# An attention and feed-forward kernel on one core: raw keys transposed two heads at a time and placed by transfers, reciprocals sent through DRAM, an order of work written out per tile, and a rearranged end of the attention part

## The chip, the cores and the metric

One core of a Trainium2 chip runs the whole kernel. The metric is the time of one execution on the device in microseconds (us), lower is better. The core has five engines with queues of their own: PE (TensorE, matmuls and transposes), ACT (ScalarE), DVE (VectorE), POOL (GpSimd) and SP (SyncE, which here issues the transfers). They wait for each other on semaphores only.

## The reference

The inputs are float32: q, k, v of 4 batches x 8 heads x 1152 rows x 64; weights of two feed-forward blocks. In attention two neighbouring query rows are averaged, so that a head has 576 query rows and 1152 keys.

```python
def _attn_ref(q, k, v):
    q_pool = q.reshape(B, H, S // 2, 2, D).mean(axis=3)
    scores = np.matmul(q_pool, k.transpose(0, 1, 3, 2)) / sqrt(D)
    attn = np.exp(scores - np.max(scores, axis=-1, keepdims=True))
    attn = attn / (np.sum(attn, axis=-1, keepdims=True) + 1e-09)
    return np.matmul(attn, v)
def _moe_ref(x, w_in, w_out):          # x: 2304 x 512, w_in: 512 x 2048
    h = x @ w_in
    g = np.where(h >= 1, h, np.where(h <= -1, 0.0, (h + 1) ** 2 / 4))
    return g @ w_out
def _moe2_ref(x, w1, w2, w3, w_out):   # 512 x 768 each
    return np.maximum(np.maximum(x @ w1, x @ w2), x @ w3) @ w_out
```

## The kernel before, in words

**Attention** goes over 16 pairs of heads, each in 9 tiles (`TILES`) of 128 query rows; the middle one (`M_TILE`) holds the last 64 rows of both heads. To keep float32 precision, operands are split into a high part (hi, rounded to the matmul's type fp32r) and a low part (lo, the rest), and products are added. Keys lie in `kT` with hi on 64 partitions and lo on the other 64, so one matmul with a doubled query sums both parts.

For a tile s these steps follow one another. *S*: PE writes scores in three groups of 384 keys (`tile_scores`), two matmuls a group (four in the middle tile), into a ring of four PSUM banks, `SCORE_RING`; a group waits (`exp_done`) until the exp of the tile that had the bank is done. *M*: DVE takes the maximum of each group, and of the three (`tile_max`). *E*: ACT makes exp in two instructions, of one and two groups (`tile_exp`). *T*: PE transposes the probabilities in three groups of three 128x128 blocks (`tile_transposes`) into a ring of three banks, `RING`. ACT copies each as pT_hi (`hi_of_tile`), DVE subtracts for pT_lo (`lo_of_tile`), which frees the bank. *V*: PE multiplies by the values in four parts a pair (n = 0 to 3: head and half), of 18 products of 288 columns each (`value_products`); the last two parts are finished in the first tiles of the next pair. ACT copies their own 64 rows to `X` and the other 64 to `value_aux`, and POOL adds them (`add_values`).

Beside that the next pairs are prepared (`PREP`). POOL splits the keys of a head into hi and lo side by side (`keys`), PE transposes 18 blocks a pair (K, six groups) and ACT copies them to `kT`. POOL adds the query pairs, PE transposes 9 blocks (Q), ACT and DVE make hi and lo. For the reciprocals of the sums (R), POOL spreads them over blocks, PE transposes five, and DVE multiplies `X` by them (`scale_x`).

The order on PE, ACT and DVE is the same row of steps in each tile: `PE_ORDER`, `ACT_ORDER` and `DVE_ORDER`, with X for the preparations of that tile. E, M and S with a number act on the next tile, N0 on the tile after it. On SP, `loads` issues the transfers of values, queries and keys, all in one queue.

**Feed-forward** goes over tiles of 384 tokens; PE makes hidden chunks (hid) and adds their products (acc), POOL splits weights into slots (`split_weights`). Three slots lie in memory that attention frees early, and are split before the last additions (`early_weights`).

## Time and profile before

| | |
|---|---|
| median of 3 runs | 1293.17 us (1292.39 to 1294.75) |
| the profiled execution | 1294.91 us, span of its trace 1293.0 us |
| granted TensorE clock, mean | 0.996 of full speed |
| busy of the span | PE 97%, DVE 59%, ACT 51%, POOL 26% |
| attention, first to last scores matmul | 12.74 to 568.22 us |
| first product of the feed-forward part's second matmul | 590.07 us |

Busy times are those of the profile; for PE they are modelled, since matmuls overlap. An idle time with an arrow names what ended it. "x3" means three instructions merged into one row.

### The profile page before, as it was taken

How to read it: one execution, taken by the hardware profiler on the slowest of the kernel's cores; microseconds unless marked ns; L12 is line 12 of the kernel's file. 1: busy time of each engine (PE TensorE's matmuls, PEld its weight loads, DVE VectorE, ACT ScalarE, POOL GpSimd, SP SyncE). 2: the span in 40 equal slices, each digit the busy share in tenths (PEclk: the TensorE clock that was granted, in tenths of full speed). 3: DMA queues.
4: the chain of work that ended last, by engine and by line, in shares of the span. 5: the costliest groups of instructions: out<-in, count | busy, mean ns of one | idle time of the engine just before them, and what ended most of it. 6: DMA issues, size and time to landing. Idle time of an engine off the chain costs nothing.

```text
span 1293.0 us, 21136 instructions
## 1 busy us (share of the span) xinstructions
PE 1259.6 (97%) x7876; PEld 1207.9 (93%) x7876; DVE 758.1 (59%) x1579; ACT 658.8 (51%) x1570; POOL 335.5 (26%) x332
## 2 busy tenths in 40 slices
PE   7999999999999999989999999999999999999998
PEld 6989899999989898979999999999999999999997
DVE  5888888888888888874544444444453222223221
ACT  5989899999989898962222222222222111111111
POOL 5343443444433444258600000000282000000000
PEclk9999999999999999989999999999999999999999
DMA  3111111111111111113300000000030000000000
GB/s 119 47 56 56 52 33 57 53 41 56 56 47 56 56 56 38 52 49 100 113 1 1 1 1 1 1 1 1 17 122 26 1 25 25 1 25 5 20 25 25
DMA packets 59140, 49.07 MB, mean 38 GB/s; under 512 B 2977, under 2 KB 48033, under 8 KB 59041
## 3 DMA queue, kind: packets, MB, share of 16 engines
q1 hardware_dynamic: 59040, 47.72, 12.1%
q8 instruction: 65, 1.06, 0.3%
q14 instruction: 35, 0.28, 0.1%
HBM read 42.99 MB, written 4.72 MB: 37 GB/s over the span
## 4 chain that ended last, share of the span: by engine, by line
PE 79%; ACT 18%; DVE 1%; issue 1%; POOL 1%; DMA 0%; SPq 0%; POOLq 0%; ACTq 0%
PE hid L868 33%; PE acc L900 16%; ACT probs L558 8%; PE trans L413 8%; ACT pT_hi L548 6%; PE acc L932 6%; PE scores L456 6%; PE values L475 5%; PE scores L458 4%; ACT kT L568 1%; ACT value_aux L582 1%; PE trans L424 1%; DVE qT L662 1%; ACT X L578 1%; ACT qT L571 1%
## 5 line engine op out<-in xcount | busy, mean ns | idle before, releaser
L626 DVE TENSOR_REDUCE neg_max_parts<-scores 128x1 f32<-128x384 f32 x432 | 234.7, 552 | 44.0 <-PE scores L458 30.3
L548 ACT ACTIVATE pT_hi<-trans 128x384 fp32r<-128x384 f32 x432 | 191.2, 491 | 55.8 <-PE trans L413 52.3
L640 DVE TENSOR_TENSOR pT_lo<-trans,pT_hi 128x384 fp32r<-128x384 f32 x432 | 212.0, 546 | 7.3 <-ACT pT_hi L548 6.3
L558 ACT ACTIVATE probs<-scores,neg_max 128x768 f32<-128x768 f32 (+1 forms) x288 | 212.0, 753 | 4.0 <-DVE neg_max L633 4.0
L456 PE MATMUL scores<-kT,qT 128*128 128x384 f32 x480 | 199.6, 416 | 9.4 <-ACT probs L558 9.1
L413 PE MATMUL trans<-ident,probs 128*128 128x128 f32 x1296 | 189.7, 273 | 9.6 <-DVE qT L662 6.4
L413 PEld LDWEIGHTS trans<-ident,probs 128*128 128x128 f32 x1296 | 157.5, 140 | 24.9 <-DVE qT L662 11.5
L868 PE MATMUL hid<-qT,w_slots 128*128 128x384 f32 x936 | 171.6, 336 | 0.0
L868 PE MATMUL hid<-x_hi,w_slots 128*128 128x384 f32 x624 | 167.6, 335 | 0.0
L868 PEld LDWEIGHTS hid<-qT,w_slots 128*128 128x128 f32 x936 | 163.7, 188 | 1.0
L986 ACT ACTIVATE excess<-rise,halves 128x384 f32<-128x384 f32 x96 | 59.2, 617 | 203.0 <-DVE rise L1070 203.0
L458 PE MATMUL scores<-kT,qT 128*128 128x384 f32 x480 | 162.2, 338 | 0.0
L900 PE MATMUL acc<-own_g,w_slots 128*128 128x384 f32 x648 | 143.1, 336 | 0.0
L900 PEld LDWEIGHTS acc<-own_g,w_slots 128*128 128x128 f32 x648 | 115.6, 188 | 0.0
L868 PEld LDWEIGHTS hid<-x_hi,w_slots 128*128 128x128 f32 x624 | 113.7, 188 | 0.6
L456 PEld LDWEIGHTS scores<-kT,qT 128*128 128x128 f32 x480 | 91.6, 191 | 23.4 <-ACT probs L558 20.1
L339 POOL TENSOR_TENSOR X<-X,value_aux 64x288 f32<-64x288 f32 x64 | 51.2, 799 | 221.8 <-ACT value_aux L582 220.4
L1084 DVE TENSOR_TENSOR excess<-hid,rise 128x384 f32<-128x384 f32 x36 | 20.1, 557 | 147.5 <-PE hid L868 147.5
L868 PE MATMUL hid<-x_lo,w_slots 128*128 128x384 f32 x312 | 104.6, 335 | 0.0
L475 PE MATMUL values<-pT_hi,v_split 128*128 128x288 f32 x576 | 95.7, 297 | 0.9 <-ACT value_aux L582 0.9
L980 ACT ACTIVATE k_split<-hid 128x384 fp32r<-128x384 f32 x66 | 32.5, 492 | 121.8 <-DVE hid L1087 77.1
L1070 DVE TENSOR_SCALAR rise<-hid 128x384 f32<-128x384 f32 x96 | 53.4, 556 | 68.0 <-PE hid L868 67.8
(101 smaller groups left out, 1998.2 us busy)
## 6 DMA issues: line engine op xcount, KB each, us to landing
k_raw<-in_k SPq DMA_DIRECT2D x16, 576.0 KB, 4.0
v_raw<-in_v SPq DMA_DIRECT2D x32, 288.0 KB, 2.8
q_raw<-in_q SPq DMA_DIRECT2D x32, 256.0 KB, 3.0
out<-X SPq DMA_DIRECT2D x18, 256.0 KB, 2.8
q_raw<-in_moe_w_out SPq DMA_DIRECT2D x14, 256.0 KB, 3.1
k_raw<-in_moe_w SPq DMA_DIRECT2D x12, 256.0 KB, 3.1
k_raw<-in_moe_w_in SPq DMA_DIRECT2D x8, 256.0 KB, 2.9
k_raw<-in_moe_w_out SPq DMA_DIRECT2D x8, 256.0 KB, 3.0
```

The lines of the kernel that those rows point to most:

```text
L413: last = pe.transpose(trans[:, bank, j * P:(j + 1) * P], probs[:, par, at:at + P], ident[:])
L456: pe.matmul(scores[:, bank, 0:SB], qT_hi[:, qp, cols], kT[:, qp, h, keys], start=(m == 0), stop=False)
L458: last = pe.matmul(scores[:, bank, 0:SB], qT_lo[:, qp, cols], kT[:, qp, h, keys], start=False, stop=(m == len(terms) - 1))
L475: last = pe.matmul(values[:, 0:HALF], v_split[:, h, kt].rearrange("p a d -> p (a d)"), pT[part][:, h, kt, half * HALF:(half + 1) * HALF], ...
L548: act.activation(*tile_places(pT[0], src, t, g), ACT.Copy).then_inc(p_hi_done, 1)
L558: act.activation(probs[:, par, :].rearrange("p (n k) -> p n k", n=GROUPS)[:, ns[0]:ns[-1] + 1], scores[:, bank:bank + len(ns), 0:SB], ACT. ...
L626: dve.tensor_reduce(neg_max_parts[:, par, n:n + 1], scores[:, score_banks(u9)[n], 0:SB], AX_X, ALU.max, negate=True).then_inc(parts_done, 1)
L640: dve.tensor_tensor(*tile_places(pT[1], src, t, g), hi.bitcast(F32), ALU.subtract).then_inc(p_lo_done, 1)
L868: last = pe.matmul(out_bank, weight(slot, part, half, k), x[par][:, k, :], start=(k == 0 and part == 0 and x is x_hi), stop=(k == KC - 1 a ...
L900: last = pe.matmul(acc[:, m, 0:NT], weight(f, part, 1, m), g[f % 2], start=(f == 0 and n == 0), stop=(f == C1 - 1 and n == 2))
L932: last = pe.matmul(acc[:, sub, :], g[f % 2][:, sub * P:(sub + 1) * P], w_slots[2 * f + 1][:, part, HALF_W:2 * HALF_W], start=(f == 0 and n ...
L986: act.activation(squares[:], clamped[:], ACT.Square, bias=halves[:, 0:1], scale=0.5).then_inc(square_done, 1)
```

## The change

The kernel computes the same. In each part:

- Keys (from the second pair on): the raw keys of two heads lie side by side in `k_raw`; PE transposes 9 blocks (three groups), ACT copies hi and DVE subtracts lo, both into `k_parts`, and SP places the four quarters in `kT` with transfers from SBUF to SBUF. The first pair is prepared as before, by DVE.
- Reciprocals: SP stores the 1152 numbers in DRAM and loads them back spread over 64 partitions; POOL multiplies `X` by them (`scale`).
- Values: ACT copies all 128 rows in one instruction to one half of `value_all`, SP moves 64 rows to the other partitions (`move_values`), POOL adds.
- Order: three tables name each step with its tile within the pair. H is ACT's pT_hi, L is DVE's pT_lo, W is a product of the pair before.
- End: 8 weight slots instead of 3 are split before the last scaling, in another order, and the hi part of the first token tile is made by ACT.

```diff
-PREP = {0: [("K", 0)], 1: [("K", 1)], 2: [("K", 2)], 3: [("K", 3)], 4: [("K", 4), ("R", 0)],
-        5: [("K", 5)], 6: [("R", 1), ("Q", 0), ("Q", 1), ("Q", 2)]}
-PE_ORDER = ["S1", "T0", "S2", "T1", "T2", "N0", "V", "X"]
-ACT_ORDER = ["T0", "T1", "T2", "E0", "E1", "X", "V"]
-DVE_ORDER = ["T0", "T1", "T2", "M0", "X", "M1", "M2"]
+T5.0 T5.1 V0:8-13 V0:13-18 S7.0 T5.2 S7.1 S7.2
...
+H5.0 H5.1 E6.0 E6.1 V0 H5.2
...
+L5.0 L5.1 M7.0 M7.1 M7.2 L5.2
...
+            for h in range(2):
+                src = k_heads[bass.ds(head(pair) + h, 1)].rearrange("h p (t d) -> p (h t) d", d=D)
+                sp.dma_start(k_raw[:, :, h, :], src).then_inc(k_loaded, 16)
...
+        def place_k(pair):
+
+            sp.wait_ge(k_lo_done, pair * KG)
+            for h in range(2):
+                for a in range(2):
+                    copy_parts(sp, kT[rows_of(a), pair % 2, h, :], k_parts[rows_of(h), a, :], k_placed)
+
+        def send_recips(pair):
+
+            sp.wait_ge(recip_done, pair + 1)
+            sp.dma_start(recip_rows[pair % 2].rearrange("(t p) -> p t", p=P), recips[:],
+                         allow_slow_non_contiguous=True).then_inc(recip_sent, 16)
...
+        def move_values(pair, n):
+
+            done = pair * 4 + n
+            h = n // 2
+            sp.wait_ge(value_kept, done + 1)
+            if done >= 1:
+                sp.wait_ge(add_done, done)
+            sp.dma_start(value_aux[rows_of(h), :], value_all[rows_of(1 - h), n % 2, :]).then_inc(value_moved, 16)
...
+        for i in range(PAIRS):
+            if i > 0:
+                send_recips(i - 1)
+            load_v(i, 1)
+            if i > 0:
+                move_values(i - 1, 2)
+            if i + 1 < PAIRS:
+                place_k(i + 1)
+                if i + 2 < PAIRS:
+                    load_k(i + 2)
+            if i > 0:
+                spread_recips(i - 1)
+                move_values(i - 1, 3)
+            if i + 1 < PAIRS:
+                load_v(i + 1, 0)
+                if i + 2 < PAIRS:
+                    sp.wait_ge(q_trans_done, (i + 1) * QG)
+                    load_q(i + 2)
...
+            move_values(i, 0)
+            move_values(i, 1)
...
+        for i in range(PAIRS):
+            head_values(i, 0)
...
+            if i > 0:
+                add_values(i - 1, 2, (v_ready, 2 * i + 1))
+            head_values(i, 1)
+            if i > 0:
+                add_values(i - 1, 3, (v_ready, 2 * i + 2))
+                scale(i - 1)
+            if i + 2 < PAIRS:
+                queries(i + 2)
+            if i == PAIRS - 1:
+                split_weights(0)
+            add_values(i, 0)
+            if i == PAIRS - 1:
+                split_weights(1)
+            add_values(i, 1)
+        add_values(PAIRS - 1, 2, split_weights(2))
+        add_values(PAIRS - 1, 3, split_weights(3))
+        for n in range(4, 8):
+            split_weights(n)
+        scale(PAIRS - 1)
...
+        def key_transposes(pair, g):
+
+            group = ("K", pair, g)
+            wait_bank(group)
+            pe.wait_ge(k_loaded, 32 * (pair + 1))
+            for j in range(GK):
+                src = k_raw[:, g * GK + j].rearrange("p h d -> p (h d)")
+                last = pe.transpose(trans[:, BANK[group], j * P:(j + 1) * P], src, ident[:])
+            last.then_inc(k_trans_done, 1)
...
+        def keep_values(pair, n):
+
+            done = pair * 4 + n
+            act.wait_ge(value_done, done + 1)
+            if done >= 2:
+                act.wait_ge(add_done, done - 1)
+            act.activation(value_all[:, n % 2, :], values[:, 0:HALF], ACT.Copy).then_inc(value_kept, 1)
...
+        def keys(pair, g):
+
+            dve.wait_ge(k_hi_done, (pair - 1) * KG + g + 1)
+            cols = slice(g * GK * P, (g + 1) * GK * P)
+            dve.tensor_tensor(k_parts[:, 1, cols], trans[:, BANK["K", pair, g], 0:GK * P],
+                              k_parts[:, 0, cols].bitcast(F32), ALU.subtract).then_inc(k_lo_done, 1)
...
+    def early_high(act):
+
+        act.wait_ge(*ends["scaled"]((KC - 1) * 4 + 1))
+        act.wait_ge(*ends["scores_done"])
+        act.activation(x_hi[0], x_tiles[:, :, 0:NT], ACT.Copy).then_inc(x_hi_done, 1)
```

PE in tile 5 of a pair in the middle, before. L456 and L458 are the two matmuls of a score group (S), L413 the transposes of probabilities (T), L475 value products, L424 key transposes:

```order
L456 MATMUL scores<-kT,qT 128x384
L458 MATMUL scores<-kT,qT 128x384
L413 MATMUL trans<-ident,probs 128x128 x3
L456 MATMUL scores<-kT,qT 128x384
L458 MATMUL scores<-kT,qT 128x384
L413 MATMUL trans<-ident,probs 128x128 x6
L456 MATMUL scores<-kT,qT 128x384
L458 MATMUL scores<-kT,qT 128x384
L475 MATMUL values<-pT_hi,v_split 128x288
L475 MATMUL values<-pT_lo,v_split 128x288 x9
L424 MATMUL trans<-ident,k_split 128x128 x3
```

PE in the same tile now (L491 and L492 are S, L427 is T, L508 are value products):

```order
L427 MATMUL trans<-ident,probs 128x128 x6
L508 MATMUL values<-pT_hi,v_split 128x288
L508 MATMUL values<-pT_lo,v_split 128x288 x9
L491 MATMUL scores<-kT,qT 128x384
L492 MATMUL scores<-kT,qT 128x384
L427 MATMUL trans<-ident,probs 128x128 x3
L491 MATMUL scores<-kT,qT 128x384
L492 MATMUL scores<-kT,qT 128x384
L491 MATMUL scores<-kT,qT 128x384
L492 MATMUL scores<-kT,qT 128x384
```

The transposes of the tile now come first, and the two score groups that wait for this tile's exps come last; they belong to tile 7 (two ahead), where before they belonged to tile 6.

ACT in tiles 5 and 6 of a pair in the middle, before (L548 is pT_hi, L558 exp, L568 a key copy, L578 and L582 the two value copies):

```order
L548 ACTIVATE pT_hi<-trans 128x3x128 x3
L558 ACTIVATE probs,sums<-scores,neg_max 128x768
L558 ACTIVATE probs,sums<-scores,neg_max 128x384
L568 ACTIVATE kT<-trans 128x384
L578 ACTIVATE X<-values 64x288
L582 ACTIVATE value_aux<-values 64x288
L548 ACTIVATE pT_hi<-trans 128x3x128 x3
L558 ACTIVATE probs,sums<-scores,neg_max 128x768
L558 ACTIVATE probs,sums<-scores,neg_max 128x384
```

And now (L557 is exp, L603 the value copy, L569 a query copy):

```order
L548 ACTIVATE pT_hi<-trans 128x3x128 x2
L557 ACTIVATE probs,sums<-scores,neg_max 128x768
L557 ACTIVATE probs,sums<-scores,neg_max 128x384
L603 ACTIVATE value_all<-values 128x288
L548 ACTIVATE pT_hi<-trans 128x3x128 x3
L557 ACTIVATE probs,sums<-scores,neg_max 128x384
L569 ACTIVATE qT<-trans 128x2x64
L557 ACTIVATE probs,sums<-scores,neg_max 128x768
```

One of the three pT_hi copies of a tile now stands behind both exps, and a single value copy stands for two.

## Rows read from the trace of the kernel before

**Rows 1.** Timeline, DVE: start, length in us, engine, line, operation, names
```profile
303.25 0.21 DVE L675 RECIPROCAL recips<-safe_sums 128x9 f32<-128x9 f32 x1
...
373.18 0.21 DVE L675 RECIPROCAL recips<-safe_sums 128x9 f32<-128x9 f32 x1
```
**Rows 2.** Window of two pairs: length, busy PE, PEld, DVE, ACT, POOL, clock, DMA, GB/s
```profile
303.25:373.18 69.93, 67.88 (x492) 63.85 (x492) 61.14 (x142) 62.92 (x162) 29.45 (x34) 1.00 0.17 52
```
**Rows 3.** Chain that ended last, last pair, in order of time: start, us, what
```profile
548.95 0.44 PE scores L456
549.39 0.18 PE scores L458
...
550.25 0.34 PE trans L413 x3
...
550.61 0.88 ACT pT_hi L548 x2
551.49 0.89 ACT probs L558 x2
...
552.42 0.44 PE scores L456
...
562.48 1.32 PE values L475 x10
...
567.10 0.44 PE scores L456
...
568.22 0.19 PE scores L458
...
568.60 1.05 POOL qT L835
...
569.73 2.38 POOL qT L837
```
**Rows 4.** Groups by form in the window of rows 2: busy us, mean ns, idle before
```profile
L626 DVE TENSOR_REDUCE neg_max_parts<-scores 128x1 f32<-128x384 f32 x54 | 29.4, 552 | 5.6 <-PE scores L458 3.8
L640 DVE TENSOR_TENSOR pT_lo<-trans,pT_hi 128x384 fp32r<-128x384 f32 x54 | 26.5, 545 | 0.4 <-ACT pT_hi L548 0.3
...
L339 POOL TENSOR_TENSOR X<-X,value_aux 64x288 f32<-64x288 f32 x8 | 6.4, 800 | 26.8 <-ACT value_aux L582 26.6
L568 ACT ACTIVATE kT<-trans 128x384 fp32r<-128x384 f32 x12 | 6.1, 508 | 0.0
...
L582 ACT ACTIVATE value_aux<-values 64x288 f32<-64x288 f32 x8 | 3.2, 405 | 0.2
...
L648 DVE TENSOR_TENSOR X<-trans,X 128x512 f32<-128x512 f32 x2 | 1.4, 686 | 0.0
...
L653 DVE TENSOR_TENSOR X<-trans,X 64x64 f32<-64x64 f32 x4 | 0.9, 217 | 0.0
```
**Rows 5.** Page, DMA issues: names, count, size, median us from issue to landing
```profile
k_raw<-in_k SPq DMA_DIRECT2D x16, 576.0 KB, 4.0
v_raw<-in_v SPq DMA_DIRECT2D x32, 288.0 KB, 2.8
```
**Rows 6.** Timelines of SP, DVE and POOL at the start
```profile
0.80 0.45 SPq L253 DMA_DIRECT2D k_raw<-in_k  x1
...
5.22 0.75 DVE L703 CAST k_split<-k_raw 128x576 fp32r<-128x576 f32 x1 [5.22 <-DMA k_raw<-in_k]
...
7.17 1.40 POOL L317 TENSOR_TENSOR q_raw<-q_raw 128x576 f32<-128x576 f32 x1 [4.87 <-DMA q_raw<-in_q]
```
**Rows 7.** Window at the start, columns as in rows 2
```profile
4.00:5.00 1.00, 1.00 (x7) 1.00 (x6) 0.00 (x0) 0.00 (x0) 0.00 (x0) 1.00 1.13 348
```
**Rows 8.** Timeline, PE, end of attention; in brackets idle before and what ended it
```profile
574.56 0.90 PE L413 MATMUL trans<-ident,probs 128*128 128x128 f32 x3 [2.81 <-DVE pT_lo L640]
...
580.71 1.47 PE L475 MATMUL values<-pT_hi,v_split 128*128 128x288 f32 x9 [0.92 <-ACT value_aux L582]
...
590.07 0.44 PE L900 MATMUL acc<-k_split 128*128 128x384 f32 x1
```

More of the change, by code:

```diff
@@ L144, in prep_of, with ring_order @@
-    def prep_of(u, t, first, last):
-        return [(kind, g) for kind, g in PREP.get(t, [])
-                if not (kind == "R" and first and u == 0) and not (kind in "KQ" and last and u == 1)]
-    def group_count(kind, pair, t, g):
+    WARM_UP, BRIDGE = 22, 10
+    FIRST = [("FK", 0), ("FK", 1), ("FK", 2), ("FQ", 0)]
+    SECOND = [("FK", 3), ("FK", 4), ("FK", 5), ("FQ", 1), ("FQ", 2)]
+    def ring_order():
+        groups = FIRST + SECOND
+        for pair in range(PAIRS):
+            for step in steps_of(PE_ORDER):
+                if step[0] == "T":
+                    groups.append(("T", pair * TILES + step[1], step[2]))
+                elif step[0] in "KQ" and pair + 1 < PAIRS:
+                    groups.append((step[0], pair + 1, step[1]))
+        return groups
@@ new lines, in tile_scores @@
+        def tile_scores(s, n):
+            pair, t, qp = s // TILES, s % TILES, (s // TILES) % 2
+            if n == 0 and t == 0 and pair > 0:
+                pe.wait_ge(k_placed, 64 * pair)
+                pe.wait_ge(q_lo_done, pair * QG)
+            if n == 0 and s == 0:
+                pe.wait_ge(first_k_done, 3)
+                pe.wait_ge(first_q_lo, 1)
+            if n == 0 and t == M_TILE:
+                if pair == 0:
+                    pe.wait_ge(first_k_done, 6)
+                    pe.wait_ge(first_q_lo, 3)
+            before = bank_before(s, n)
+            if before is not None:
+                pe.wait_ge(exp_done, before)
+            out = scores[:, score_banks(s)[n], 0:SB]
+            keys = slice(n * SB, (n + 1) * SB)
@@ L447, in tile_scores, with value_products @@
                 terms = [(2 + t if t < M_TILE else 1 + t, HEAD_OF[t])]
[L448 to L466 removed]
+            for m, (blk, h) in enumerate(terms):
+                cols = slice(blk * P, (blk + 1) * P)
+                pe.matmul(out, qT_hi[:, qp, cols], kT[:, qp, h, keys], start=(m == 0), stop=False)
+                last = pe.matmul(out, qT_lo[:, qp, cols], kT[:, qp, h, keys], start=False, stop=(m == len(terms) - 1))
+            last.then_inc(scores_done, 1)
+        def value_products(pair, n, products):
+            h, half = n // 2, n % 2
+            t = (2, M_TILE, 7, TILES - 1)[n]
             for m in products:
@@ L528, in pe_program @@
-        two_pairs(0, first=True)
-        for d in range(1, PAIRS // 2 - 1):
-            two_pairs(d)
-        two_pairs(PAIRS // 2 - 1, last=True)
-        for half in range(2):
-            start = VALUE_STEPS[TILES - 1][2].stop if half == 0 else 0
-            value_products(PAIRS - 1, 1, half, range(start, 2 * KT))
-        meanwhile(0)
-        for g in range(RG):
-            bank, before = RING_END[g]
-            wait_bank(before, PAIRS - 2)
-            prep_transposes(PAIRS, 0, "R", g, bank)
@@ new lines, in dve_program @@
+        for kind, g in FIRST:
+            first_rest(kind, g)
+        for n in range(GROUPS):
+            tile_max(0, n)
+        for kind, g in SECOND:
+            first_rest(kind, g)
+        for n in range(GROUPS):
+            tile_max(1, n)
+        for pair in range(PAIRS):
+            for step in steps_of(DVE_ORDER):
+                kind = step[0]
+                if kind == "L":
+                    lo_of_tile(pair * TILES + step[1], step[2])
+                elif kind == "M" and pair * TILES + step[1] < ALL_TILES:
+                    tile_max(pair * TILES + step[1], step[2])
+                elif kind == "K" and pair + 1 < PAIRS:
+                    keys(pair + 1, step[1])
+                elif kind == "Q" and pair + 1 < PAIRS:
+                    queries(pair + 1, step[1])
+                elif kind == "R" and pair > 0:
+                    reciprocals(pair - 1)
@@ L942, in two_tiles1 @@
                 for f in range(C1):
-                    if not (first and u == 0 and f < EARLY):
-                        hidden1(pe, tile, f, u)
+                    hidden1(pe, tile, f, u)
                     if f >= LAG1:
```

848 lines of the change are left out of this document (375 added, 473 removed).

## The prediction

> **What bounds the kernel now.** First the period of a pair of heads: DVE's eighth and tenth reciprocals start 69.93 us apart, 34.97 us a pair [rows 1]. Then the busy times of these two pairs: DVE 61.14 us and ACT 62.92, or 30.6 and 31.5 a pair, at a granted clock of 1.00; PE 67.88, or 97% [rows 2]. PE's is a modelled time, in which matmuls overlap, so I rebuild its work from the distances between starts. The chain that ended last has them: a scores matmul that follows another takes 0.18, three transposes 0.34, ten value products 1.32 [rows 3]. A pair has 60 scores matmuls (10.5 us at 0.175), 81 transposes of probabilities (8.9 at 0.11), 72 value products (9.5 at 0.132), and 18 transposes of keys, 9 of queries and 5 of reciprocals (2.0, 1.0 and 0.55). Together 32.4 us. So no engine fills the 34.97; 2.5 us a pair are lost to dependences.
>
> The chain shows which. From 548.95 to 552.42 it makes one full round [rows 3]: first scores matmul after a wait (0.44 instead of about 0.18), the rest of S1, T0, S2, T1, T2 on PE, then ACT's last two pT_hi copies (0.88), then the first exp (0.89), which frees the bank for the next S1. That is 3.47 us a tile, because ACT's exp of tile s+1 stands behind all three pT_hi copies of tile s, and those behind PE's scores. Nine such rounds are 31.2 us, and key, query and value copies lengthen some. The last pair has no keys or queries: its scores restarts at 548.95 and 567.10 are five tiles, 3.63 a tile, 32.7 a pair [rows 3]. Taking away 27 transposes (3.0 us) with their copies gave only 2.3. So the order matters as much as the work.
>
> **The change, part by part.**
>
> *Keys.* PE transposes 9 raw blocks (two heads side by side) instead of 18: -9 x 0.11 = -1.0 us a pair. ACT copies 3 groups instead of 6: -3 x 0.51 = -1.5 [rows 4]. DVE gets 3 subtractions of the shape of pT_lo, 0.545 each alone and about 0.5 behind each other: +1.5 [rows 4]. POOL loses two splits and has room.
>
> *Reciprocals.* PE -5 x 0.11 = -0.55. DVE loses 0.69 and two of 0.22: -1.1 [rows 4]. They go to POOL and DMA.
>
> *Values.* ACT makes 4 copies of 128 partitions instead of 8 of 64. Both have 288 columns, so I take 0.405 each: -1.6 [rows 4].
>
> Floors a pair: **PE 32.4 - 1.5 = 30.9; DVE 30.6 - 1.1 + 1.5 = 31.0; ACT 31.5 - 1.5 - 1.6 = 28.4**. ACT, which carried the old round, gets the most room, and DVE, on no old chain, becomes a bound beside PE.
>
> *The order.* The new rows put each tile's scores a whole tile earlier for most of the pair, and one pT_hi copy behind the exps. The round is now exp (0.89), two score groups on PE (0.44 + 0.18 + 0.35, and about 0.17 for the last to drain), the last maximum (0.55), neg_max (about 0.2) and the gaps of the semaphores: 2.9 us a tile, 26 a pair. It lies below the floors, so the period goes by them plus in-order waits. What remains is a restart price: a scores matmul after a wait costs 0.27 more than one behind another (0.44 against about 0.17) [rows 3]. I keep five of those in nine tiles, 1.4 us, and get **32.4 us a pair**. The bounds are 31.5 (two of them) and 33.4 (all nine, 2.4). Gain 2.57 (1.5 to 3.5) for each of the 15 pairs that prepare a next one: **-38.5 us** (-22 to -52). The last pair's floor is PE's 30.9 - 1.0 - 1.0 = 28.9, with 1.4 more 30.3, from 32.7: **-2.4** (-1.5 to -3).
>
> *What covers the new transfers.* SP now issues, in one queue, the reciprocals out and back (4), four placements of 64 x 1152, four moves of values, two key loads instead of one, beside the old value and query loads. The trace has no SBUF to SBUF transfer and no store of 4-byte elements. From below they are bounded by the 2.8 us in which a value load lands, from above by twice the 4.0 of a key load [rows 5]. Keys are last written in tile 2 and read by S9.0 in tile 7: five tiles, about 18 us, against four issues and a landing, 5 to 10. Raw keys are loaded from tile 3 for tile 0 of the next pair: six tiles. Nothing on PE waits. The tightest cover is that of values: ACT's W2 copy at the end of tile 0 waits for POOL's first addition of that pair. POOL reaches it after queries, whose load SP sends only after Q2, tile 6. From there: four issues of 0.45, a landing of 2.8, two passes over the queries of at most 1.40, an addition of 0.80 [rows 4 to 6]: 8.2 us against some 3.5 tiles, 12.5. Cover 4.3 us; when it is gone each microsecond stops ACT, and behind it exp, scores and PE. Cost taken: nothing, with its own rival below.
>
> *The start.* First keys land at 5.22; queries start at 7.17 as soon as their load lands, and this load is on the chain [rows 6]. Both streams together move at 348 GB/s [rows 7]. Keys go from runs of 2304 bytes to 256, and SP issues one more transfer (0.45) ahead of the queries. If a packet costs what its bytes cost, +0.5; if 256 bytes cost as much as 512, the keys' 590 KB take 3.4 instead of 1.7 us: +2.2; at twice that again, +5.6. I take **+2**. The Trainium skill, "DMA: Bandwidth & Descriptors", Specifications, puts line rate at 512 bytes and more, and says that smaller ones are read, modified and written. It speaks against this change; no row here has a transfer of that size to check it. By it the start would cost about the 2.2 or more, and the sum stays within 4 us of mine; by full rate at 256 bytes the sum would be 1.5 lower.
>
> *The end.* From the last scores matmul (568.22) to the first acc (590.07) are 21.9 us [rows 3, 8]. After it PE's instructions are the same in both, and I change nothing there. PE's work in it: 46 value products 6.1, 9 transposes 1.0, 5 of reciprocals 0.55, 36 hidden matmuls 6.3: 14 us. 8 are lost: POOL's third weight split (1.05 + 2.38) stands before the addition for which ACT waits, and PE waits 2.81; a further 0.92 for value_aux; and three transposes at 574.56 take 0.90 [rows 3, 8]. Now no copy waits behind that split, the copy of values is one, and x_hi is made by ACT. I leave 2.5 us of waits (ACT's 128x1536 copy of X, 1.8 us by twice the exp of half its length, ahead of the W2 copy, and the last exp): **-5.5** (-2 to -7). If the third weight split, now behind the last value product, were later than two hidden groups (4.2 us), PE would wait; it needs 3.4, so it does not.
>
> **Sum** on the profiled execution, 1294.9 us (its span is 1293.0): -38.5 - 2.4 - 5.5 + 2.0 = -44.4, so 1250.5. The median of the runs, 1293.2, is 1.7 lower: **1249 us**. Own range, with all terms at one end: 1232 to 1274.
>
> **Rivals.**
> 1. *The old round stays.* In-order waits keep exp behind copies, and work only falls: the last pair turned 3.0 us of PE work into 2.3, so 1.5 give 1.2 a pair, -18; with the other terms 1269. For it: the old loss was all waits. Against: the new S and exp rows. 0.14.
> 2. *DVE becomes the bound with its own waits.* Its order interleaves maxima and pT_lo, each waiting on PE or ACT. With 3 us of waits on 31.0 the period is 34.0: -15, in all 1273. 0.10.
> 3. *The floors are reached.* Period 31.0: -60, in all about 1228. 0.08.
> 4. *Slower: the values chain.* The addition for W2 comes late through query load, POOL and SP. Place: ACT in tile 0. Up to 4.3 us late it costs nothing. It decides from about 7.3 us (4.3, the gain of 2.57, and the 5.9 of the other terms over 15 pairs); at 8 us late a pair costs 32.4 + 3.7 = 36.1, +17, in all near 1304. What could make it so late is the queue: 1152 elements of 4 bytes and two key loads of 256-byte runs go ahead of the moves. By the rule of the Trainium skill named under the start, both would be slow. 0.06.
> 5. *Nothing is gained*: an unseen wait takes it all, within 0.2%. 0.04, part of it on the slower side.
>
> Forecast 0.58. A measurement of this kernel tells about 0.2% (2.6 us) from no change. Faster 0.90, same 0.03, slower 0.07. The range 1236 to 1276 holds nearly all of the forecast and of rivals 1 and 2, and leaves out rivals 3 to 5 and the tips: under 2 in 10.
>
> **What would show it.** Right: reciprocals 32 to 33 us apart; DVE busy near 31 a pair and 95% of it, ACT under 29; no long row with ACT value_all waiting for POOL; DVE's first split of keys 1 to 4 us later than 5.22; the first acc about 16 us after the last score. Wrong: ACT idle in tile 0 behind POOL; PE waiting for the placement of keys in tile 7; a round in the chain that still passes scores, three pT_hi copies and exp; key loads of over 10 us.

## The result

The changed kernel took 1273.95 us, median of 4 runs (1272.43 to 1275.53), beside 1292.85 of the kernel before (1292.39 to 1294.75): a ratio of 0.985, 95% interval 0.984 to 0.986. That is 18.9 us faster; 44 were forecast. The profiled execution has a span of 1273.4 us against 1293.0, so 19.6 us less. In two later sets, each on a chip of its own beside the kernel before, the same kernel took 1290.8 us (1287.7 to 1295.9) and 1292.3 (1290.3 to 1295.5), almost the time of the kernel before (ratio 0.999 both times). Both things have to be explained: why 19 and not 44, and why at other times nearly nothing.

Four stretches give the whole difference of the spans. They are cut at three marks: the first reciprocal of the program, the fifteenth, and the first acc matmul.

| stretch | before | after | measured | forecast |
|---|---|---|---|---|
| start and pair 0, to the first reciprocal | 57.98 | 58.11 | +0.1 | -0.6 |
| 14 periods | 489.70 | 462.39 | -27.3 | -36.0 |
| fifteenth reciprocal to first acc | 42.39 | 39.36 | -3.0 | -7.9 |
| first acc to the end | 702.9 | 713.5 | +10.6 | 0 |

The forecast's gain of 2.57 a pair belongs to 15 pairs: pair 0, in the first stretch beside the +2.0 of the start (-0.6 together), and the 14 of the second. The third has only the last pair and the end, -2.4 and -5.5.

The new DVE row has the reciprocals ahead of the maxima, behind three pT_lo, and they come some 1.9 us earlier in a tile (an estimate from the rows). So +0.1 and -3.0 are really about +2.0 and -4.9. Cut instead at DVE's maximum for the first tile of a pair, which both kernels make in tile 7 of the pair before, the four are +1.5, -26.7, -5.0 and +10.6.

The page of the changed kernel, busy time of the engines:

```profile
PE 1235.9 (97%) x7661; PEld 1182.5 (93%) x7661; DVE 757.6 (59%) x1575; ACT 613.8 (48%) x1462; POOL 277.2 (22%) x240
```

PE is at 97% of the span, but in that number a late restart looks like work, so the periods say more. Windows of the 14 periods, before and after, columns as in [rows 2]:

```profile
57.98:547.68 489.70, 475.20 (x3430) 446.76 (x3429) 427.80 (x994) 440.58 (x1121) 202.02 (x234) 1.00 0.16 49
```
```profile
58.11:520.49 462.38, 449.59 (x3233) 420.38 (x3231) 427.49 (x994) 399.03 (x1024) 151.35 (x153) 1.00 0.61 106
```

PE's busy time, restarts included, fell by 25.6 us and its idle time by only 1.7 (from 14.5 to 12.8). DVE's reciprocals (timeline: start, length) stood 34.97 us apart [rows 1]:

```profile
256.11 0.22 DVE L703 RECIPROCAL recips<-safe_sums 128x9 f32<-128x9 f32 x1
287.87 0.21 DVE L703 RECIPROCAL recips<-safe_sums 128x9 f32<-128x9 f32 x1
322.38 0.21 DVE L703 RECIPROCAL recips<-safe_sums 128x9 f32<-128x9 f32 x1
355.36 0.22 DVE L703 RECIPROCAL recips<-safe_sums 128x9 f32<-128x9 f32 x1
```

The periods are 31.76, 34.51 and 32.98; all 14 have a mean of 33.03. Three windows of one pair each, columns as in [rows 2]:

```profile
322.38:355.36 32.98, 31.98 (x232) 30.06 (x232) 30.46 (x72) 28.50 (x74) 10.88 (x11) 1.00 0.63 109
355.36:387.46 32.10, 32.02 (x232) 30.03 (x231) 30.40 (x72) 28.39 (x74) 9.52 (x10) 1.00 0.67 112
287.87:322.38 34.51, 32.30 (x232) 29.84 (x230) 30.86 (x72) 28.82 (x74) 12.30 (x13) 1.00 0.59 105
```

In the second PE is busy for all but 0.08 us: this is PE's floor as the rows show it, near 32, and a pair of 34.51 has the same work and 2.2 us of waits. DMA's share is 0.6, from 0.17 [rows 2]. Where PE waits in the slow pair the timeline of ACT and PE shows (in brackets idle before and what ended it):

```profile
303.14 0.49 ACT L548 ACTIVATE pT_hi<-trans 128x384 fp32r<-128x384 f32 x1 [0.34 <-PE trans L427]
...
303.58 0.60 ACT L577 ACTIVATE qT<-trans 128x512 fp32r<-128x512 f32 x1
...
304.07 0.90 ACT L557 ACTIVATE probs<-scores,neg_max 128x768 f32<-128x768 f32 x1
...
305.11 0.44 PE L491 MATMUL scores<-kT,qT 128*128 128x384 f32 x1 [1.21 <-ACT probs L557]
```

The exponential of two banks stands behind a pT_hi copy and a copy of queries, and PE's next scores wait 1.21 us for the bank that it frees. Such waits for an exponential, of 0.44 to 1.21 us, come about every fourth tile (289.23, there of a transpose, 305.11, 319.17, 334.63). The scores turn through four banks in threes; where a tile's three lie in banks 3, 0 and 1 (every fourth tile), the exponentials are of one and two banks in place of two and one, and the second, of two, comes late in ACT's row.

The end, timeline of SP, POOL and PE:

```profile
554.65 0.59 SPq L279 DMA_DIRECT2D recip_rows<-recips  x1
...
558.65 0.47 SPq L302 DMA_DIRECT2D k_split<-value_all  x1
...
564.16 0.47 SPq L289 DMA_DIRECT2D k_split<-recip_rows  x1
...
569.52 0.79 POOL L369 TENSOR_TENSOR X<-value_all,k_split 64x288 f32<-64x288 f32 x1 [7.14 <-DMA k_split<-value_all]
...
574.10 2.29 PE L888 MATMUL hid<-qT,w_slots 128*128 128x384 f32 x6 [7.22 <-POOL w_slots L860]
```

The first acc stands at 559.86, 30.2 us earlier than before [rows 8]. But the store of the last pair's reciprocals, 1152 elements of 4 bytes, is issued at 554.65, and the spread, which waits for its landing, at 564.16: 9.5 us. The last move of values, issued behind it, takes 10.7 us to POOL; POOL's weight splits stand behind that addition, and PE waits 7.22 us for the fifth. What the 16 DMA engines recorded in that time (windows; the last two numbers are their busy share and GB/s):

```profile
555.00:558.00 3.00, 3.00 (x19) 2.99 (x19) 1.12 (x2) 0.76 (x2) 2.71 (x3) 1.00 0.31 26
558.00:561.00 3.00, 3.00 (x19) 3.00 (x18) 1.59 (x3) 1.28 (x3) 2.64 (x3) 1.00 0.01 4
561.00:564.00 3.00, 2.69 (x16) 2.37 (x15) 1.59 (x3) 1.28 (x3) 1.38 (x1) 1.00 0.16 19
564.00:567.00 3.00, 2.87 (x17) 2.56 (x15) 1.68 (x3) 0.66 (x3) 0.00 (x0) 1.00 0.60 140
```

The store's own packets stand before 558. Then, with two weight loads and the move issued (557.59 to 558.65), the engines record almost nothing for three microseconds and little for three more: the others wait, and no engine looks busy. What holds them there is not shown.

The other 3.4 us of the 10.6 go largely to the clock. (1.1 to 1.2 of the 10.6 stay in every kernel below whose store has longer runs, 704.0 to 704.1 us from the first acc on, and are not the store's.) Windows from the first acc on:

```profile
559.86:574.10 14.24, 6.70 (x38) 6.07 (x37) 4.39 (x8) 2.90 (x6) 6.66 (x6) 0.84 0.44 99
```
```profile
574.00:620.00 46.00, 45.90 (x248) 45.91 (x249) 20.69 (x32) 11.08 (x20) 41.07 (x24) 0.94 0.43 138
```

PE idles for half of the first, and behind that its granted clock is 0.94 over 46 us of unbroken work: for 12% of them, 5.5 us, it was at the lower level of 1.2 GHz, which costs 2.8 us (46 times 0.06).

DMA issues of the page, columns as in [rows 5]:

```profile
kT<-k_split SPq DMA_DIRECT2D x60, 288.0 KB, 5.9
k_raw<-in_k SPq DMA_DIRECT2D x32, 288.0 KB, 6.9
```

A load of half the bytes takes 6.9 us in place of 4.0. At the start (timeline of DVE and POOL):

```profile
5.87 0.49 DVE L709 CAST k_split<-k_raw 128x576 fp32r<-128x576 f32 x1 [5.87 <-DMA k_raw<-in_k]
...
7.90 1.70 POOL L347 TENSOR_TENSOR q_raw<-q_raw 128x576 f32<-128x576 f32 x1 [5.61 <-DMA q_raw<-in_q]
```

Keys come 0.65 us and queries 0.73 us later than in [rows 6].

### The profile page after: what moved, and what is told of

The parts are those of the page before. It is cut to its first block, busy times and chain, and to the rows that moved or that the text cites. A ratio compares the mean times of both kernels' runs of the same rounds, so it can differ in the third digit from the quotient of the medians.

```text
span 1273.4 us, 20668 instructions
## 1 busy us (share of the span) xinstructions
PE 1235.9 (97%) x7661; PEld 1182.5 (93%) x7661; DVE 757.6 (59%) x1575; ACT 613.8 (48%) x1462; POOL 277.2 (22%) x240
## 2 busy tenths in 40 slices
DMA packets 124610, 76.26 MB, mean 60 GB/s; under 512 B 62560, under 2 KB 111712, under 8 KB 124512
## 3 DMA queue, kind: packets, MB, share of 16 engines
q1 hardware_dynamic: 124512, 74.94, 29.8%
## 4 chain that ended last, share of the span: by engine, by line
PE 90%; ACT 3%; DVE 2%; DMA 2%; issue 1%; POOL 1%; SPq 0%; POOLq 0%; DVEq 0%; ACTq 0%
PE hid L888 32%; PE acc L916 16%; PE trans L427 11%; PE values L508 11%; PE scores L491 7%; PE scores L492 6%; PE acc L948 6%; ACT probs L557 2%; DMA k_split<-value_all 1%; PE trans L437 1%; PE trans L447 1%; ACT pT_hi L548 1%; DVE neg_max_parts L637 1%; DVE pT_lo L651 0%; DVE X L1100 0%
## 5 line engine op out<-in xcount | busy, mean ns | idle before, releaser
L637 DVE TENSOR_REDUCE neg_max_parts<-scores 128x1 f32<-128x384 f32 x432 | 230.9, 551 | 22.4 <-PE scores L492 19.5
L548 ACT ACTIVATE pT_hi<-trans 128x384 fp32r<-128x384 f32 x432 | 199.6, 494 | 68.7 <-PE trans L427 65.8
L651 DVE TENSOR_TENSOR pT_lo<-trans,pT_hi 128x384 fp32r<-128x384 f32 x432 | 221.1, 549 | 5.6 <-ACT pT_hi L548 4.2
L557 ACT ACTIVATE probs<-scores,neg_max 128x768 f32<-128x768 f32 (+1 forms) x288 | 213.6, 744 | 7.4 <-DVE neg_max L644 5.9
L491 PE MATMUL scores<-kT,qT 128*128 128x384 f32 x480 | 188.2, 392 | 12.5 <-ACT probs L557 12.2
L427 PE MATMUL trans<-ident,probs 128*128 128x128 f32 x1296 | 196.0, 274 | 3.2 <-ACT probs L557 1.8
L427 PEld LDWEIGHTS trans<-ident,probs 128*128 128x128 f32 x1296 | 156.7, 141 | 22.9 <-DVE pT_lo L651 9.6
L492 PE MATMUL scores<-kT,qT 128*128 128x384 f32 x480 | 163.6, 341 | 0.0
L369 POOL TENSOR_TENSOR X<-value_all,k_split 64x288 f32<-64x288 f32 x64 | 52.9, 826 | 308.4 <-DMA k_split<-value_all 306.0
L491 PEld LDWEIGHTS scores<-kT,qT 128*128 128x128 f32 x480 | 91.6, 191 | 25.4 <-ACT probs L557 23.0
L508 PE MATMUL values<-pT_hi,v_split 128*128 128x288 f32 x576 | 105.1, 309 | 0.9 <-ACT value_all L603 0.5
L508 PE MATMUL values<-pT_lo,v_split 128*128 128x288 f32 x576 | 100.3, 301 | 0.0
```

What stands on the lines that cost most here:

```text
L427: last = pe.transpose(trans[:, BANK[group], j * P:(j + 1) * P], probs[:, s % 2, at:at + P], ident[:])
L491: pe.matmul(out, qT_hi[:, qp, cols], kT[:, qp, h, keys], start=(m == 0), stop=False)
L492: last = pe.matmul(out, qT_lo[:, qp, cols], kT[:, qp, h, keys], start=False, stop=(m == len(terms) - 1))
L508: last = pe.matmul(values[:, 0:HALF], v_split[:, h, kt].rearrange("p a d -> p (a d)"), pT[part][:, h, kt, half * HALF:(half + 1) * HALF], ...
L548: act.activation(*tile_places(pT[0], src, s % TILES, g), ACT.Copy).then_inc(p_hi_done, 1)
L557: act.activation(probs[:, par, :].rearrange("p (n k) -> p n k", n=GROUPS)[:, ns[0]:ns[-1] + 1], scores[:, bank:bank + len(ns), 0:SB], ACT. ...
```

## The experiments

Each set of runs was made on one chip, beside the kernel before (1293.1 to 1293.6 in all of them).

### First set: the end, the order, the store

**The store on ACT's queue.** Only the last pair's store of reciprocals moves from SP to ACT.

```
-        send_recips(PAIRS - 1)          # SP, behind move_values(.., 2)
+        act.wait_ge(recip_done, PAIRS)  # ACT, behind early_high
+        act.dma_start(recip_rows[..].rearrange("(t p) -> p t", p=P), recips[:], ...)
```

> The changed kernel with one edit: the last pair's store of reciprocals is issued on ACT's transfer queue instead of SP's, between the two weight loads. Theory A (the 1152 elements of 4 bytes hold up SP's queue for some 9 us, and the last value move stands behind them): the last move lands in 3 to 4 us instead of 10.71, PE's wait of 7.22 us for the fifth weight split goes, and with it the 2.1 us of slow clock: 10 us less than the changed kernel. Theory B (the move is late because of the two weight loads, 0.5 MB, ahead of it in the queue): it still takes about 10 us, and less than 2 us is gained.

Measured: 1280.6 us (1278.1 to 1282.5), ratio 0.990. The stall at the end stayed. Timeline:

```profile
561.33 0.47 SPq L302 DMA_DIRECT2D k_split<-value_all  x1
572.35 0.79 POOL L368 TENSOR_TENSOR X<-value_all,k_split 64x288 f32<-64x288 f32 x1 [7.60 <-DMA k_split<-value_all]
...
576.93 3.57 PE L890 MATMUL hid<-qT,w_slots 128*128 128x384 f32 x10 [7.61 <-POOL w_slots L862]
```

The move on SP's queue still needs 11 us, with the store on another queue. So the store need not stand in SP's queue to delay the move: the two share something behind their queues. This run alone doesn't rule out theory B, the two weight loads ahead of the move, since both its time and its stall are as B has them; the store in rows below does. There the same loads stand ahead (551.81 and 552.24), the move is issued at 552.88, and POOL adds it at 556.82 without waiting for it. That the whole is 6.6 us above 1273.95 says little of the edit, as the later sets showed.

**Exponentials together.** In the tiles with parts of one and two banks, ACT makes the second exponential right behind the first.

```
+            for t in range(1, TILES + 1):
+                if len(exp_parts(pair * TILES + t)[0]) == 1:
+                    steps.remove(("E", t, 1))
+                    steps.insert(steps.index(("E", t, 0)) + 1, ("E", t, 1))
```

> The changed kernel with one edit: in each tile whose scores lie in banks 3, 0, 1 (every fourth tile; there the first exp is of one group and the second of two) ACT's second exp stands directly behind the first, not behind a pT_hi, query or value copy. Theory C (PE's waits of 0.34 to 1.21 us, one in four tiles, come from that copy in between; they make the pairs 31.8 to 34.7 us long in a pattern of four): the pattern shrinks, the mean of 33.0 falls to about 32.4, 6 to 10 us less in all. Theory D (the waits come from the maxima on DVE, or move elsewhere): less than 3 us.

Measured: 1270.6 us (1269.7 to 1272.7), ratio 0.983, mean period 32.79. This is 3.3 us less than the changed kernel's first time, between theory C (6 to 10) and theory D (under 3), on a chip where the loads land later (8.2 us); the third set shows more. PE's waits for exponentials fall to 2.9 us in the 14 pairs from 10.6, and no period lies at 34.5 for that reason; one of 34.09 has another: there ACT waits 1.96 us for POOL's addition, and PE behind it 1.56.

**The old rows.** The three tables get the old fixed order; the work stays the changed kernel's.

> The changed kernel with its work, transfers and end, but with the three tables filled with the fixed rows of the kernel before (S1 T0 S2 T1 T2 S0 of the tile after, values, preparations; three pT_hi copies and then both exps; three pT_lo and then the maxima), queries all in tile 6. Theory E (the old round of 3.47 us a tile bounds it, the order is worth as much as the work): the period of a pair is 33.8 us or more against 33.0, and 10 to 14 us are lost against the changed kernel. Theory F (only the work counts): within 3 us of the changed kernel.

Measured: 1295.7 us (1292.3 to 1298.4), ratio 1.002, mean period 34.46, keys landing after 10.9 us. It is 21.7 us over 1273.95, where theory E had 10 to 14. Read alone, this says that the work brings nothing and the order all. The last set corrects it.

**The store in rows.** Every pair's store writes 128 runs of 36 bytes instead of 1152 elements of 4. The numbers then lie in another order, so X is scaled with other reciprocals; nothing else changes.

```
-            sp.dma_start(recip_rows[pair % 2].rearrange("(t p) -> p t", p=P), recips[:],
+            sp.dma_start(recip_rows[pair % 2].rearrange("(p t) -> p t", p=P), recips[:],
```

> The changed kernel, but all stores of reciprocals write 128 rows of 36 bytes instead of 1152 elements of 4, so that the numbers lie in another order in DRAM and the scaling uses wrong ones; all else is the same. Theory A: the last store lands in about 3 us instead of 9.5, the last value move in 3 to 4, PE's wait of 7.22 is gone: 10 us less than the changed kernel, and the pairs before are as long as before (their cover holds). If the pairs too get shorter, the stores cost there as well, which nobody expects.

Measured: 1260.1 us (1259.6 to 1260.5), ratio 0.974. The stores land in 1.7 us (median of the 16), nothing waits at the end, and from the first acc it takes 704.1 us, as before the change (702.9). The waits for exponentials stay (1.22 us at 170.34, 0.79 at 200.21).

### Second set: can it be avoided?

**The order of ACT and DVE alone, in the kernel before.**

```
-ACT_ORDER = ["T0", "T1", "T2", "E0", "E1", "X", "V"]
+ACT_ORDER = ["T0", "T1", "E0", "T2", "E1", "X", "V"]
-DVE_ORDER = ["T0", "T1", "T2", "M0", "X", "M1", "M2"]
+DVE_ORDER = ["T0", "T1", "M0", "T2", "X", "M1", "M2"]
```

> The kernel before, with nothing of the change but the order inside a tile: ACT makes T0 T1 E0 T2 E1 in place of three copies ahead of the exponentials, DVE T0 T1 M0 T2 in step. Theory G (the order alone loosens the old round, in which the first exponential stands behind three copies that wait for PE's transposes): the pair falls from 34.98 to 33.0 to 33.8 us, so 1261 to 1275 us for the whole. Rival H (the order pays only together with the work that the change takes off PE and DVE): within 3 us of the kernel before, 1290 to 1296 us. Between the two, each has its share as the period shows.

Measured: 1300.2 us (1300.1 to 1300.4), ratio 1.006, mean period 35.44 from 34.98. Neither theory. Exp ahead of the third copy, with PE's order unchanged, makes the old kernel slower.

**The last store late.** The weight slot over the spread reciprocals is used thirteenth in place of ninth; SP issues the last store behind nine weight loads and the spread behind three more, and POOL's splits go on meanwhile.

> The changed kernel with one weight slot (the one that lies over the spread reciprocals and the values' second half) used as the thirteenth in place of the ninth, so that the last pair's store of reciprocals can be issued behind eight weight loads and after the last move of values. Theory A (the store of 1152 elements of 4 bytes holds every DMA engine and so makes the last value move late): the wait of 7.2 us near the first output product shrinks to under 1 us and the time falls by 7 to 11 us to 1263 to 1267 us. Rival I (the store only changes places: it now makes the weight loads late, and PE waits for POOL's splits later on): 1271 to 1276 us with a wait of 4 us or more for w_slots some 20 to 50 us further on.

Measured: 1284.2 us (1283.0 to 1289.0), ratio 0.994. Timeline of SP, POOL and PE:

```profile
584.01 0.43 SPq L279 DMA_DIRECT2D recip_rows<-recips  x1
...
586.94 3.61 SPq L831 DMA_DIRECT2D q_raw<-in_moe_w_out  x1
...
599.31 2.60 POOL L862 TENSOR_SCALAR w_slots<-q_raw 128x1024 fp32r<-128x1024 f32 x1 [8.85 <-DMA q_raw<-in_moe_w_out]
...
604.38 4.21 PE L892 MATMUL hid<-qT,w_slots 128*128 128x384 f32 x12 [7.21 <-POOL w_slots L864]
```

The stall of 7.2 us has moved 30 us on with the store: now a weight load is held up, and POOL and PE behind it. This is rival I by its mechanism; the time is 8 us above rival I's range. A store of this kind has to be paid wherever loads are short of cover.

**The store in rows, with the full output.** DVE turns the reciprocals in blocks of 32 x 32 (one more instruction a pair), and the store is four transfers of nine runs of 128 bytes.

```
-            sp.dma_start(recip_rows[pair % 2].rearrange("(t p) -> p t", p=P), recips[:], ...)
+            rows = recip_rows[pair % 2].rearrange("(t b c) -> b t c", b=4, c=32)
+            for b in range(4):
+                sp.dma_start(rows[b], recips_t[32 * b:32 * b + TILES, :])
...
+            dve.transpose(recips_t[:], recips[:]).then_inc(recip_done, 1)
```

> The changed kernel with the reciprocals turned by one DVE transpose of 32 x 32 blocks ahead of the store, so that each store is four transfers of nine runs of 128 bytes in place of one of 1152 elements of 4 bytes; the output is the full one. Theory A (what costs is the number of elements in the store): the store lands in about 2 us, no wait over 1 us at the end, and the time falls by 11 to 15 us, as with the earlier kernel that stored 36-byte rows: 1259 to 1263 us. Rival (the four issues and the DVE operation take back part of it): 1264 to 1270 us.

Measured: 1262.6 us (1261.9 to 1264.1), ratio 0.977. The page of this kernel, its packets (and of the changed kernel's page: 124610 packets, 62560 under 512 B, q1 29.8%), and two DMA issues:

```profile
DMA packets 107074, 76.26 MB, mean 61 GB/s; under 512 B 45024, under 2 KB 94176, under 8 KB 106976
...
q1 hardware_dynamic: 106976, 74.94, 23.5%
...
kT<-k_split SPq DMA_DIRECT2D x60, 288.0 KB, 4.6
k_raw<-in_k SPq DMA_DIRECT2D x32, 288.0 KB, 5.6
```

The bytes are the same. The share of the 16 engines falls by 6.3 points of the span, some 83 us of all 16. By the size of the packets in the two traces this isn't the time of the small elements themselves: packets of 4 bytes take 12.3 us of all 16 engines in the changed kernel and 3.9 here, 0.5 us a store, while the same 5120 packets of 2304 bytes take 114.4 and 43.8, a mean of 358 ns and 137. With the store, other transfers' packets take longer. Key loads and placements land 1.3 us sooner although nothing in them changed.

**The first keys in long runs.** Only pair 0's keys are loaded in runs of 2304 bytes.

```
+                if pair == 0:
+                    sp.dma_start(first_raw[:, h, :], k_heads[..].rearrange("h p n -> p (h n)"))
```

> The changed kernel with only the first pair's keys loaded in runs of 2304 bytes, as before; every later pair's stay at 256 bytes. Theory J (the start's loss is the short runs): the first keys land 0.6 us sooner, queries 0.7 us sooner, the first exponential 0.7 to 1.2 us sooner, and the whole is 0.7 to 1.2 us shorter, 1272.8 to 1273.3 us beside 1274. Rival K (the start's loss is PE's clock or another chain): first exponential within 0.2 us of the changed kernel's 16.47 us, no difference in time.

Measured: 1280.3 us (1279.1 to 1284.0), ratio 0.990. Keys are there at 4.54 us and queries at 6.74 in place of 5.87 and 7.90, so the start is as foreseen, but the whole was 6 us more than 1273.95. In the pairs there are periods of 36.34, 35.18 and 35.53. Since the edit touches nothing there, the question was whether the changed kernel itself would give 1274 again.

### Third set: the changed kernel again

The first kernel is the changed one with no edit; the second is the last one above; the third has the row store and the exponentials together; the fourth has all three edits.

> The changed kernel itself, once more. The last kernels that kept the store of 4-byte elements took 1280 and 1284 us though their edits should have cost nothing. Theory L (with that store the values' transfers come late by an amount that differs from run to run and from chip to chip): this run lies off 1274 by several us, 1270 to 1281, with the difference in pairs of 35 us and more in which POOL waits over 10 us for a value's transfer. Rival M (the edits themselves cost what was seen): 1273 to 1275 us as before.

> The changed kernel with the first pair's keys in runs of 2304 bytes, beside the changed kernel of the same chip. Theory L: within 2 us of it, a little less (0.5 to 1.5). Rival M: 6 us more than it.

> Row stores (32 x 32 transpose of the reciprocals on DVE) and the two exponentials back to back in the tiles whose scores begin in bank 3 ... 0 (every fourth tile). Separately they gave 1262.5 and 1270.6. Theory N (the two losses are apart): with the store gone the wait for the value's adding goes too, so that the exponentials' gain shows whole: pair 32.4 to 32.6 us instead of 32.99, 1254 to 1258 us. Rival O (the gain of one is taken back by DVE's waits for ACT's copies): 1260 to 1264 us, pair 32.9.

> The same with the first pair's keys in runs of 2304 bytes: first exponential 0.7 to 1.2 us sooner and as much off the whole, 1253 to 1257 us (theory J); rival K: no difference from the kernel without it.

| kernel | median (range), us | mean of 14 periods | keys' landing |
|---|---|---|---|
| changed | 1290.8 (1287.7 to 1295.9) | 34.37 | 8.8 |
| changed, first keys long | 1288.5 (1286.4 to 1290.8) | 33.99 | 8.4 |
| row store, exps together | 1251.8 (1250.7 to 1252.8) | 32.32 | 5.7 |
| all three | 1250.9 (1250.4 to 1251.0) | 32.30 | 5.6 |

The changed kernel is 17 us slower than in the result, farther than its expectation's range. The timeline of SP, POOL, ACT and PE in its pair of 37.96 us (125.56 to 163.52) shows how:

```profile
127.27 0.38 SPq L279 DMA_DIRECT2D recip_rows<-recips  x1
...
131.88 0.47 SPq L302 DMA_DIRECT2D k_split<-value_all  x1
...
141.83 0.81 POOL L369 TENSOR_TENSOR X<-value_all,k_split 64x288 f32<-64x288 f32 x1 [10.42 <-DMA k_split<-value_all]
...
148.00 0.54 SPq L302 DMA_DIRECT2D k_split<-value_all  x1
...
152.98 0.79 POOL L369 TENSOR_TENSOR X<-value_all,k_split 64x288 f32<-64x288 f32 x1 [7.84 <-DMA k_split<-value_all]
...
153.86 0.41 ACT L603 ACTIVATE value_all<-values 128x288 f32<-128x288 f32 x1 [3.37 <-POOL X L369]
...
155.36 0.91 PE L508 MATMUL values<-pT_hi,v_split 128*128 128x288 f32 x5 [3.19 <-ACT pT_hi L548]
```

The move of W2, issued 4.6 us behind the store, is added 10 us later; SP gets the move of W3 out only at 148.00, and POOL adds it at 152.98. Only then may ACT keep V1, in tile 7: it waits 3.37 us, an exponential and pT_hi copies stand behind that, and PE's value products wait 3.19 us for them. Theory L has the direction and the long pairs with POOL's waits of over 10 us; its stated range was too narrow. POOL waits 296 us for values' transfers in the result's run and here alike, so nearly all of that costs nothing. The time in which ACT waits for POOL, between 60 and 550 us, is 9.1 here and 0.2 there. It is only part of the difference: the 14 periods are 18.8 us longer, PE idles 25.4 us in them in place of 12.8 (its scores wait for exponentials 15.3 us between 60 and 550 us, from 10.6), and their mean granted clock is 0.989 in place of 1.000, which costs 5.1 us.

With the store in rows, the exponentials' edit brings 10.8 us (1262.6 to 1251.8, on different chips), theory N and somewhat more. The window of one pair of the third kernel:

```profile
312.76:345.24 32.48, 32.17 (x231) 29.76 (x230) 30.46 (x73) 28.35 (x74) 10.34 (x11) 1.00 0.45 111
```

PE waits 0.2 us for exponentials in 14 pairs, from 9.1 in the row store's kernel. The first keys' long runs bring 2.4 us beside the changed kernel and 0.9 beside the other, within the spread of the runs both times. In the fourth kernel queries are there at 6.78 us against 8.03, but the clock from 10 to 16 us was 0.77 against 1.00, and the first exponential came 0.28 us sooner. What the short runs cost at the start is so 1.1 to 1.3 us to the queries, and what of it reaches the end isn't settled.

### Fourth set: order and work again, without the store

> The kernel with the row store, and with the three tables of the order put back to the old fixed rows. The earlier run of the old rows (1295.7) still had the store of 4-byte elements, whose price differs from run to run. Theory E (the order is worth about 20 us by itself): 1278 to 1286 us beside 1262 of the row store with the new order. Theory F (the work alone brings most of it and the store hid that): 1265 to 1272 us.

> The row store with the new order once more, the yardstick of this set. Theory L (only kernels with the 4-byte store differ from run to run): 1261 to 1264 us again, its keys landing after 5.6 us. Rival P (all kernels with this many transfers do): off by over 4 us.

> The changed kernel a third time (1273.9 and 1290.8 so far). Theory L: anywhere from 1272 to 1292 us, and the pair's mean period and the landing of the keys (6.9 us at 1273.9, 8.8 us at 1290.8) go with it. Rival M: within 2 us of one of the two, with the landing of the keys unrelated.

| kernel | median (range), us | mean of 14 periods | keys' landing |
|---|---|---|---|
| row store, old order | 1279.7 (1278.9 to 1280.9) | 34.23 | 5.5 |
| row store, new order | 1262.6 (1261.4 to 1263.6) | 32.92 | 5.5 |
| changed | 1292.3 (1290.3 to 1295.5) | 34.14 | 8.6 |

The row store gives 1262.55 on both of its chips, the changed kernel 1273.95, 1290.8 and 1292.3 in its three sets. On this one chip the 4-byte store costs 29.7 us: by the marks above, 17.1 in the 14 periods, 2.2 to the first acc, 10.5 after it. And the change's halves come apart, with the 4-byte store out of both: the work brings 13.9 us (1293.6 to 1279.7), the order 17.1 more. "Work" here is all that isn't order, the rearranged end included: of its gain 10.5 us lie in the 14 periods. Of the order's 18.3 us in the periods, 10.5 are idle time of PE (22.1 to 11.6) and 7.8 its busy time, in which restarts are counted (457.2 to 449.3).

## Why the prediction was off

The time lay inside the range and 25 us above the forecast. The direction was right; the amount was less than half. Point by point:

**Transfers: "Cost taken: nothing".** This is the step that failed most: a term put at nothing that was 10.6 us at the end in the result's run, and with what it did to the pairs nearly 30 us at other times. The store of 4-byte elements was bounded by twice a key load's 4.0 us, 8; it took 9.5 at the end, so the bound was near. What I did not price is that it delays every other transfer, those of other queues too, and I looked for its effect only where values cover it in the middle of the program. At the end of attention there is no cover: +10.6 us where I had 0. "It needs 3.4, so it does not" dealt with the third weight split; PE waited for the fifth. Taking the store away gives back 11.4 us on the result's figures (1273.95 to 1262.55, from different sets), and 29.7 beside the changed kernel on one chip.

**Rival 4, the values chain,** had the right cause (the small elements ahead of the moves) and the wrong end of it: where it struck, the late addition was that of W3, and ACT waited at V1 in tile 7, not at W2 in tile 0. In the run of the result ACT waited 0.2 us, so there the rival was absent. In the two later sets the longer pairs and the end together took nearly the whole gain, but ACT's waits for POOL are 9.1 and 4.7 us, of 18.8 and 15.6 that the 14 periods grew by; what else makes PE's exponentials late there isn't shown. At 0.06 its chance was too small: its price was known to no row, and the text named both that it could be large and that its cover was 4.3 us.

**The restarts: "I keep five of those in nine tiles, 1.4 us".** The floor of 30.9 and the restarts, 32.4 together, were near: PE's busy time, in which restarts are counted, is 449.6 us in 14 periods, 32.1 each, and 32.1 again in the kernels with the row store. (The rows can't part the two terms; in the fastest pairs PE goes on without a pause for 31.8 to 32.0.) What I left out is the wait itself: I priced five restarts and no idle time, and PE idles 0.9 us a pair, in few and long waits of 0.4 to 1.2 us about every fourth tile, behind an exponential that stands too late in ACT's row. In the result's run that makes 33.03, 0.63 over my 32.4, 8.7 us in 14 periods. The period of 32.4 is what the kernel gives (32.32) once both the store and that place in the row are mended; I had read the new rows for an average tile, not for the four positions of the banks.

**Order against work.** "So the order matters as much as the work" is borne out: 17.1 us beside 13.9. The old round, however, wasn't ACT's alone: exp ahead of the third copy made the kernel before slower by 6.9 us. Whether it pays only with PE's scores a tile earlier isn't shown: the two moves weren't tried apart.

**The floors of DVE and ACT** (31.0 and 28.4) came out at 30.4 to 30.9 and 28.4 to 28.8 of busy time; rival 2 (DVE the bound) didn't come.

**Start, +2, and pair 0.** With the reciprocals' shift this stretch is about +2.0, which looks like my start term and is so by luck: pair 0's gain of 2.57 should have stood against it. The first exponential came 1.17 us later (16.47 from 15.30), by way of 0.7 us on keys and queries and a granted clock of 0.50 from 10 to 16 us, the lower level throughout, against 0.73 before; the same kernel had 1.00 there in the fourth set. From that exponential to the first reciprocal it took 41.6 us, 43.5 with the shift, beside 42.7 before, so pair 0 gained nothing. With the row store, at a clock of 1.00, it is 41.5; with the exponentials together as well, 39.3. So 2.2 us of pair 0's missing gain came back with the exponentials' edit.

The Trainium skill, "DMA: Bandwidth & Descriptors", Specifications, has full rate from 512 bytes. The trace agrees in kind: 267 GB/s from 3 to 4 us, where the trace has packets of 256 bytes, against 345 before, where most of the bytes are in packets of 2304, about three quarters. But the queries' packets of 512 bytes behind them went at 262 to 266 from 5 to 7 us, against 348 before, when nearly all were of 512 bytes [rows 7], so the size of a packet alone doesn't give its rate.

**Last pair and end, -7.9:** -4.9 after the shift, of which the store explains 1.5 of the 3.0 missing (37.86 us without it, 39.36 with it). For the rest, about 1.5 us, there is no experiment.

What stays open is why the store costs 11 us at one time and 30 at two others. The landing of the keys goes with it (6.9 us against 8.8 and 8.6; 7.9 in the three edited kernels that took 1280 to 1284), and the kernels without it agree to 0.1 us between two chips, but nothing here tells a chip's trait from where its buffers lie in memory.

## What to carry to other kernels

Count the elements of a transfer, not its bytes: 4.5 KB in 1152 pieces held up transfers of 288 KB by microseconds, on other queues too, and one small transpose on an engine with room, with the store in runs of 128 bytes, removed it. When work is moved to DMA, look for the place with the least cover (the end of a phase, where weights are due), not at the average one. When buffers turn with a period that isn't the loop's, read a hand-made order once for each position of the turn.

The best version found keeps the change and adds the row store, the exponentials together and long runs for the first keys: 1250.9 us, 3.3% less than the kernel before.

## What was unexpected in the hardware

- The landing of loads that the store has nothing to do with moved with it: 5.5 to 5.9 us for 288 KB in runs of 256 bytes without the 4-byte store, 6.9 to 8.8 with it, and 10.9 with it and the old order.
- A store of 1152 elements of 4 bytes to DRAM took 9.5 us from issue to the next dependent issue, though its packets took 0.5 us of all 16 DMA engines and those engines recorded a share of 0.01 from 558 to 561 us; as 128 runs of 36 bytes such stores landed in 1.7 us (median).
- Moving it to another engine's queue left the delay of the others as it was (11 us for a move of 72 KB, whose median landing is 2.8 to 3.0).
- The same program with that store took 1274, 1291 and 1292 us in three sets, with the kernel before within 0.8 us in all of them.
